# Slot 2's first products turned by DMA and VectorE instead of TensorE, and two block transposes moved

## The reference

```python
# 1. causal attention, 8 heads of 64, with a bias from cumulated gates
scores = scale * q @ k.T + min(-(cum_i - cum_j), 0);  attn = softmax(scores) @ v
# 2. mixture of 8 experts, one for each token
e = fresh_e if s == 0 or local_gate[b, s] < 0.5 else prev_e
h = np.maximum(x[b, s] @ w1[e], 0.0)           # 512 -> 1024
out[b, s] = p[e] * (h @ w2[e])                 # 1024 -> 512
# 3. gated convolution: h = relu(x @ w_in), gate = sigmoid(conv3(h)), (h * gate) @ w_out
```

## Time and profile before

| | before |
|---|---|
| median of 3 runs | 730.33 us (729.81 to 731.61) |
| profiled execution | 729.78 us, span 728.0 us |
| TensorE busy | 716.3 us, 98% of the span |
| VectorE busy | 458.4 us, 63% |
| ScalarE, GpSimd busy | 316.1 us (43%), 329.2 us (45%) |
| HBM | 157 GB/s over the span |
| granted TensorE clock | 1.000 |

### The profile page before, as it was taken

One profiled execution on the slowest core, in us unless ns is written; L12 is line 12 of the kernel. 1 busy time (PEld: TensorE's weight loads), 2 busy tenths in 40 slices (PEclk: granted clock), 3 DMA queues, 4 the chain that ended last, 5 costly groups with the idle time before them and its releaser, 6 DMA issues.

```text
span 728.0 us, 13518 instructions
## 1 busy us (share of the span) xinstructions
PE 716.3 (98%) x4227; PEld 590.4 (81%) x4227; DVE 458.4 (63%) x1088; ACT 316.1 (43%) x634; POOL 329.2 (45%) x442
## 2 busy tenths in 40 slices
PE   8999999999898999999999999999999999999998
PEld 6676767676687887888888888888999999899886
DVE  5778778778777445665756657575499436436610
ACT  4778778787621023222222422100687435435610
POOL 7758898988415466672737667141321100000000
PEclk9999999999999999999999999999999999999999
DMA  8888888885144768877779786722411100000011
GB/s 173 211 208 227 220 221 223 213 224 146 36 162 129 231 212 280 301 236 238 248 259 318 221 244 236 234 99 75 129 51 30 66 15 16 30 30 14 30 44 58
DMA packets 114966, 115.35 MB, mean 158 GB/s; under 512 B 63804, under 2 KB 84052, under 8 KB 114900
## 3 DMA queue, kind: packets, MB, share of 16 engines
q1 hardware_dynamic: 94372, 68.54, 32.7%
q10 hardware_dynamic: 17056, 34.69, 14.6%
q0 software_dynamic: 3472, 11.28, 5.3%
HBM read 87.14 MB, written 27.34 MB: 157 GB/s over the span
## 4 chain that ended last, share of the span: by engine, by line
PE 69%; DVE 2%; issue 1%; DMA 1%; ACT 0%; POOLq 0%; DVEq 0%; ACTq 0%
PE wide_bank L1376 18%; PE wide_bank L1706 14%; PE row_bank L1745 13%; PE row_bank L1393 10%; PE bank L1393 9%; PE bank L1342 1%; PE bank L1675 1%; DMA x_slots<-x_rows,token_of 1%; PE wide_bank L1415 0%; PE wide_bank L28 0%; PE bank L1695 0%; PE row_bank L1695 0%; DVE h_tr L1491 0%; PE bank L1029 0%; PE bank L1686 0%
## 5 line engine op out<-in xcount | busy, mean ns | idle before, releaser
L915 POOL TENSOR_TENSOR ring<-raw_w,ring 128x2048 fp32r<-128x2048 f32 x28 | 128.7, 4620 | 91.1 <-ACT ring L905 91.1
L905 ACT ACTIVATE ring<-raw_w 128x2048 fp32r<-128x2048 f32 x30 | 55.8, 1908 | 196.0 <-DMA raw_w<-in_moe_w_dram 161.6
L1706 PE MATMUL wide_bank<-x_tr,ring 128*128 128x288 f32 x768 | 107.6, 297 | 0.0
L1706 PEld LDWEIGHTS wide_bank<-x_tr,ring 128*128 128x128 f32 x768 | 103.2, 188 | 0.9
L1745 PE MATMUL row_bank<-ring,g_tr 128*128 128x512 f32 x432 | 100.2, 390 | 0.0
L690 ACT ACTIVATE prob<-score,row_min 128x128 f32<-128x128 f32 (+2 forms) x144 | 83.4, 580 | 38.4 <-PE turn_ps L362 25.6
L1745 PEld LDWEIGHTS row_bank<-ring,g_tr 128*128 128x128 f32 x432 | 80.5, 188 | 16.2
L1797 DVE SCALAR_TENSOR_TENSOR conv<-h_pad,conv_col,conv 128x576 f32<-128x576 f32 x64 | 52.2, 816 | 53.8 <-ACT conv L1858 52.5
L252 POOL TENSOR_SCALAR bias<-ncum_row,cum_col 128x128 f32<-128x128 f32 (+3 forms) x128 | 67.4, 537 | 36.7 <-DVE row_min L551 33.1
L551 DVE CUSTOM_DVE_ANT_0 score<-score_ps,bias 128x128 f32<-128x128 f32 (+2 forms) x144 | 69.2, 514 | 20.4 <-issue 13.3
L1376 PE MATMUL wide_bank<-ring,xs_tr 128*128 x312 | 74.9, 395 | 1.2 <-DVE x_slots L1507 0.8
(11 more groups left out here) (254 smaller groups left out, 1148.0 us busy)
## 6 DMA issues: line engine op xcount, KB each, us to landing
raw_w<-in_moe_w_dram ACTq DMA_DIRECT2D x12, 2048.0 KB, 11.5
x_slots<-h_turn SPq DMA_DIRECT2D x84, 128.0 KB, 3.0
ncum_row<-cum_rows SPq DMA_DIRECT2D x15, 512.0 KB, 4.9
raw_w<-in_moe_w_dram SPq DMA_DIRECT2D x12, 512.0 KB, 4.1
h_turn<-h_sb SPq DMA_DIRECT2D x11, 512.0 KB, 6.3
h_turn<-x_slots SPq DMA_DIRECT2D x10, 512.0 KB, 7.7
ncum_tail<-cum_rows SPq DMA_DIRECT2D x32, 144.0 KB, 4.3
out_dram<-out_sb ACTq DMA_DIRECT2D x18, 256.0 KB, 2.0
```

The costliest lines, as they stand in the source:

```text
L905: nc.scalar.activation(high, whole, ACT.Copy).then_inc(high_ready, 1)
L915: nc.gpsimd.tensor_tensor(low, whole, high.bitcast(F32), ALU.subtract).then_inc(low_ready, 1)
L1706: last = nc.tensor.matmul(wide_bank[j % 2][:, half, 0:HALF], ring[:, 0, w, col:col + P], x2_tr[:, x, kb, at:at + HALF], start=kb == 0 and ...
```

## The change

Slot 2 joins the slots whose first products go over DRAM (BY_PE is 2 instead of 3). TensorE no longer turns it. On SyncE's queue its write and its four reads come ahead of the store of slot 1's results. On VectorE its block transposes and moves stand between the token move of slot 5 and the relu of slot 4. The block transposes of slot 3 move from behind slot 2's results to ahead of slot 6's token move; the moves that follow them stay. The relus of slots 3 and 4 now wait for the DRAM writes of slots 2 and 3.

```diff
--- before.py
+++ after.py
@@ -1196,7 +1196,7 @@
     h_tr = sb("h_tr", [P, 2, KF, P], F32R, where=region)
     y_sb = sb("y_sb", [P, D], where=region)
     h_bank, ht_bank, x_bank, y_banks = wide_bank[0], wide_bank[1], bank[0], (row_bank[0], bank[1])
-    BY_PE = 3
+    BY_PE = 2
     BEHIND = 3
     h_swapped = [x_slots[:, 2 * n:2 * n + 2, :].rearrange("p s d -> p (s d)") for n in range(2)]
     h_other = x_slots[:, 4:6, :].rearrange("p s d -> p (s d)")
@@ -1265,9 +1265,10 @@
             sp.dma_start(y_sorted[s * P:(s + 1) * P, :], y_both[s % 2][:, :]).then_inc(y_stored[s % 2], 16)
 
         y_store(0)
-        y_store(1)
         for s in range(BY_PE, SLOTS - 1):
-            if s == 5:
+            if s == 3:
+                y_store(1)
+            elif s == 5:
                 y_store(2)
             elif s >= 7:
                 y_store(s - BEHIND - 1)
@@ -1432,8 +1433,7 @@
         turn_x(3)
         hidden(2)
         output(1)
-        turn_h(2)
-        for s in range(BY_PE, SLOTS - 1):
+        for s in range(3, SLOTS - 1):
             turn_x(s + 1)
             hidden(s)
             if s == 4:
@@ -1497,8 +1497,8 @@
                 dve.wait_ge(h_done, 2 * s + (1 + half))
                 if s > H_OTHER:
                     dve.wait_ge(h_out, 16 * (s - 1 - BY_PE))
-                elif s == BY_PE + 1:
-                    dve.wait_ge(h_out, 16)
+                elif BY_PE < s < H_OTHER:
+                    dve.wait_ge(h_out, 16 * (s - BY_PE))
                 elif s <= BY_PE:
                     dve.wait_ge(ht_turned, 2 * s if s == BY_PE else 2 * s + (half - 1))
                 to, of = h_sb[:, half * FH:(half + 1) * FH], h_bank[:, half, :]
@@ -1550,14 +1550,15 @@
         relu(2)
         move_x(3)
         move_y(1)
-        move_h(2)
         move_x(4)
         relu(3)
         move_x(5)
+        h_turned(2)
+        move_h_blocks(2)
         relu(4)
+        h_turned(3)
         move_x(6)
         move_y(2)
-        h_turned(3)
         move_h_blocks(3)
         relu(5)
         move_x(7)
```

## The result

The changed kernel takes 737.05 us (735.92 to 737.2, 4 runs) against 730.07 us (728.73 to 731.61, 4 runs) before: ratio 1.0094, interval 1.0078 to 1.0111. It is 7 us slower, and 3.7 us above the top of the range. The profiled execution took 736.92 us, span 735.1 us, against 729.78 and 728.0.

The account below looks back on a forecast made before the run. TensorE's unbroken chain was taken as the bound. The gains of 0.87 and 0.84 were swallowed by a wait for slot 3's late read, starting slot 6 1.7 later: 729.78 + 1.7 = 731.5 us, range 728.1 to 733.4.

Parts of the forecast that it names:

- the sum: TensorE from slot 6's first products: start at 279.7 against 278.0, 1.7 us later to the end, earlier gains and losses swallowed.
- part 6: Slot 3's read on SyncE's queue: last slice 0.45 behind expert 3's load, landing after 8.0 at 273.0; slot 6 starts at 279.7.
- part 3: VectorE turns slot 2: ready at 263.9, wanted by its second products at 264.55; costs nothing, 0.65 us to spare.
- part 4: Expert 2's weights before slot 5's first products: 0.9 us to spare, added traffic costs 0 to 1.2, taken as 0.
- signs of being wrong: Last slice before the load or landing below 270; TensorE waiting before slot 2's second or slot 5's first products; write after 258.
- part 1: Slot 2's eight turns removed from TensorE: -0.87 us, everything TensorE does from there comes 0.87 earlier.
- part 5: Slot 3's block transposes ahead of slot 6's token move on VectorE: -0.84 us of TensorE idle time, if the read lands by 269.6.
- A: Rival: slot 3's read gets ahead of expert 3's load, both gains stand, 728.1 us, up to 729.3; chance 0.32.
- B: Rival: slot 3's last slice goes out with the load or just ahead, lands after 6 to 7; 729.8, no change; chance 0.13.
- C: Rival: slot 2's write lands late, at 259.8, SyncE's queue comes 2.8 later; +5.4, 735.2 us; chance 0.07.

Follow-up runs that it names:

- run 1: The kernel before, with only slot 3's block transposes moved ahead of slot 6's token move: 728.45 us, ratio 0.9979.
- run 2: The changed kernel, with ScalarE's load of expert 3's first matrix held back until slot 3's reads have landed: 729.42 us, ratio 0.9993.
- run 4: The changed kernel, with slot 5's relus ahead of slot 3's block transposes and moves: 729.33 us, ratio 0.9996.
- run 3: The changed kernel, with 22 calls of matmul that nobody reads put ahead of slot 6's first products: 735.49 us, ratio 1.0085.
- run 7: The changed kernel, with 13 calls of matmul that nobody reads put ahead of slot 6's first products: 733.48 us, ratio 1.0043.
- run 10: The kernel before, with an unused write and four reads added and slot 3's block transposes ahead of slot 6's token move: 730.57 us, ratio 1.0023.
- run 8: The kernel before, with slot 5's relus ahead of slot 3's block transposes and moves: 728.91 us, ratio 0.9992.
- Run 5: The kernel before, with one unused 512 KB write to DRAM added at the place of slot 2's write: 730.04 us, ratio 1.0005.

## Why the prediction was wrong

**Right: the place, the mechanism and the sign.** Slot 2's write landed at 257.35 (said: 257.0), slot 3's reads went out at 263.94 (263.7), behind them expert 3's load at 264.40 (264.55), the read landed late, VectorE stood in front of it and TensorE idled some 3 us (3.32) before slot 6. Runs 1, 2 and 4 show each part of it: put the reads ahead of the load, hold the load back, or take the relus out of the queue, and the loss is gone.

**Wrong, the larger part: the sum,** "from 278.0 on TensorE is 279.7 - 278.0 = 1.7 us later than before" and "the delay stays as it is to the end". It took the products behind the wait at their old duration. I noted idle time of some 3 us and didn't ask what it does to the clock. The wait lowered it to half, and slot 6's products took 8.57 instead of 5.71: 2.86 us that stand in no term of the sum or of a rival. Runs 3 and 7 keep TensorE running through the wait and have the products at 5.72 and 5.75.

**Mis-sized: part 6, the landing of the read.** I took 8.0, the mean of 8.9 and 7.1, for a slice 0.45 behind the load. For such a slice that was near: the third one, 0.38 behind, took 8.9. But the last one was 0.85 behind, as the read went out 0.25 later and the load 0.15 earlier than said, and took 10.3. The time still grows there, which the rows I had, ending at 0.4, couldn't show. With 265.25 + 10.3 + 6.7 the wait ends at 282.3, 2.6 later than said. These two terms, 2.9 and 2.6, are the difference between 731.5 and 736.9.

**Mis-sized, without effect on the time: parts 3 and 4.** Both waits stand in the prediction's list of signs of being wrong. Slot 2's second products waited 0.64 for VectorE (said: nothing, 0.65 to spare), mainly since the read landed at 262.1, not at 261.3. Slot 5 waited 1.07 for weights (said: nothing): the load took 13.8, above the 13.1 that was the longest of before. As the sum said, the later wait swallows both. They are what remains in run 2, where 1.13 and 0.89 use up the gain of 1.7 from parts 1 and 5.

**The rivals.** A (the read ahead of the load) had a third of the chance, with a gain up to 1.7; in four timed runs of the changed kernel it never came. B (the slice with the load, landing after 6 to 7, the time of before) is close to what run 10 shows in another kernel: 0.06 behind the load, 7.7, a wait of 1.56 before slot 6, and a ratio that can't be told from 1. C came nearest in size (+5.4) for the wrong reason: its write lands late, here the write landed in time. The prediction read from the round robin of the Trainium skill's page "DMA: Bandwidth & Descriptors" (section "Queues, rings and completion order") that a slice behind a load would land little later than 3.0, and set it against part 6. The table is on the side of part 6: all four slices issued 0.8 or more behind a load took 10 us or more, those a microsecond or more ahead of it 3.0 to 3.3.

**Part 5 was right.** Without the exchange the early transposes remove the wait of 0.84 (run 1), and so do the early relus (run 8).

## What to carry to other kernels

Before a transfer is put ahead of work in an in-order queue, look at what else is issued around the same time: here 0.95 us, from a small read 0.10 ahead of a 2 MB load on another queue to one 0.85 behind it, made 10.3 us of landing out of 3.5. Let such a wait stand behind whatever the bottleneck engine needs next (the relus first, run 4), so that a late landing costs nothing. And where a forecast leaves the matrix engine idle for some microseconds, price the work behind it at the lower clock too, and bound the sum with that.

## What the runs showed of the hardware that was not expected

The last of the four small reads on SyncE's queue, issued 0.85 to 1.25 behind the large load of ScalarE's queue, landed 0.2 to 0.4 behind the end of that load in all four traces that have it so (changed kernel: 275.55 and 275.35). Issued 0.14 behind it, in run 4, it landed 6 us before the load did. The lag alone doesn't fix the time: behind the next load of the changed kernel (275.92) four slices issued 0.65 to 2.2 behind took 7.4 to 9.8.

The granted clock fell to 0.50 behind 4.3 us in which TensorE had 0.6 us of work. Ahead of slot 0's first products TensorE idles some 1.8 and 0.4 us in each trace, and what the clock does behind it differs: in the profiled execution of before these products took 3.00, in that of the changed kernel 4.60, with granted clocks below 0.65 from 220 to 224 (its slots had begun 1.8 earlier, so the two traces stand level again at 240, and the 7.1 above don't contain it). Run 5, which differs from before only later, has 4.48, and the other nine runs have 3.00 to 3.04. So it is a difference between executions; what decides isn't shown. The changed kernel:

```profile
218.00:220.00 2.00, 1.29 (x9) 1.13 (x10) 1.18 (x3) 1.03 (x1) 1.48 (x2) 1.00 0.36 86
220.00:222.00 2.00, 2.00 (x6) 1.61 (x6) 1.99 (x2) 0.00 (x0) 0.90 (x1) 0.53 0.62 178
222.00:224.00 2.00, 2.00 (x8) 1.55 (x7) 2.00 (x2) 0.00 (x0) 1.70 (x2) 0.61 0.00 0
```

Of the 76 executions of the kernel before that were timed beside the runs, the 13 with a mean granted clock of 0.993 lie at 730.5 to 732.3, the others at 728.5 to 730.8. The clock goes with the slow end of a kernel's spread, and doesn't explain the rest of it.
